# A two-stage feed-forward kernel: first stage in four chunks of 512 tokens and one of 256 instead of eight of 288, with shared buffers and reordered product terms

## The chip, the cores and the metric

One core of a Trainium2 chip. The metric is the device time of one execution in microseconds. Three runs of the kernel before gave 835.99, 837.09 and 838.22 us; the median is 837.09.

## The reference

2304 tokens (4 batches of 576) go through three parts:

```python
attn = softmax(block-causal(q k^T / 8)) v        # 4 batches, 8 heads, 576 x 64; blocks of 64
x = attn as [2304, 512]
h = x @ w_in                                     # [2304, 2048]
x2 = (h - tanh(h)) @ w_out                       # first FFN, [2304, 512]
do = x2 @ w_skip > 0
e = argmax(x2 @ w_gate); gate = softmax weight of e      # 8 experts
out = x2;  out[do] += gate * (relu(x2 @ w1[e]) @ w2[e])  # w1: 512 x 1024, w2: 1024 x 512
```

Every product of the two FFNs is made in float32r from a high and a low part of each operand: high x high, high x low and low x high, so three matmuls stand for one.

## The kernel before

The five engines run hand-written instruction streams that meet by semaphores. PE multiplies, ACT and DVE empty PSUM, SP and POOL issue DMAs.

**Attention** (16 pairs of heads) leaves its output transposed in `x_t`: 128 feature rows, tokens along the free axis, one stretch of 576 per head pair. Meanwhile POOL splits `w_in` into `wi_hi` and `wi_lo`; after attention it splits `w_out` (`wo_hi`, `wo_lo`).

**First FFN.** `each_chunk` (L322) runs `chunk` on PE, ACT and DVE for `NCH` = 8 chunks of `CH` = 288 tokens. In a chunk PE's `chunk` (L1335) goes over `FT` = 16 slices f of 128 hidden units. `hidden(c, f)` (L1268) is 12 matmuls (4 feature blocks x 3 terms) into one of two PSUM banks `h_ps[f % 2]`; `output(c, f-2)` (L1281) is 12 matmuls into the four banks `acc_ps`. All of them are issued by the helper `three` (L1262, so the trace shows L1265), with 128x128 weights and 288 moving columns. The order is hidden(f), output(f-2), hidden(f+1), output(f-1), and at the end output(14), output(15) with no `hidden` between.

For each f ACT takes the tanh (L698, into `tanh_h`), DVE subtracts (`g`, L966), rounds to `g_hi` (L970) and makes `g_lo` (L972). `hidden(f+2)` waits for `g` of f (its bank), `output(f)` waits for `g_hi` and `g_lo` of f. The tanh of f waits for h and for `g` of f-2. `g_hi` of f waits until output(f-2) is done. At the end of a chunk ACT rounds the next chunk's x to `x_hi` (`split_x`), DVE makes `x_lo` (L844), and ACT empties `acc_ps` into `x2_t` (L718).

**Routing of chunk c-1** lies in chunk c: on PE `logits` (12 matmuls, L1301) at f = 2, `turn_rows` (4 transposes, L1309) for the `NR` = 3 row tiles of `RT` = 96 tokens, `rank` (L1316, L1317) at f = 5; on DVE `choose` after f = 3 and `place_tokens` after f = 6. In the last chunk DVE also runs `order_experts` after f = 7 and `order_tiles` after f = 8, which make the order of the experts (`order`, L938) and the places of the first three tiles (`early_base`, L951); after L952 SP loads the first expert's weights and POOL gathers three early tiles (`rec_early`, then `xg_first` to `xg_third`, L517 to L524).

**Second FFN.** 15 tiles of 128 tokens, each of one expert. For a tile k PE runs `turn_he` (8 transposes, L1390), the `first_product` of the next tile (24 matmuls of 512 columns, moving operand `we`), `turn_gathered` (4 transposes, L1328) and `second_product` (24 matmuls of 512 columns into `y_ps`). ACT and DVE split what PE wrote into high and low (`out_xe`, `low_xe`, `out_ht`, `low_ht`). DVE's `mix` (L1058) then makes `y_rows` from `y_ps`; it waits for `y_done` and for `y_free`. There is one `y_rows`. POOL's stream for a tile is serial:

```python
            def put(k, rows):
                wait_apart(pool, y_ready, k + 2)
                pool.indirect_dma_start(out=out, ..., in_=y_rows[:], ...).then_inc(y_out, 16)
                wait_apart(pool, y_out, 16 * k + 16)
                pool.sem_inc(y_free, 1)
```

It fetches the next tile's records (L537), copies them (L542), gathers rows (L544), keeps a copy of both (L555, L556), copies the row numbers (L568), writes `y_rows` out (`put`, L560), waits until that has landed, and only then raises `y_free`. The first step of this stream waits for `base_ready`, which DVE raises at the end of `bases` (L1010).

At the seam PE runs first_product(0) for one bank, logits and turn_rows of the last chunk, the other bank, rank, and so on (L1404 to L1417); ACT and DVE have `high_pieces` and `low_first` (L1071) of the first weights between their steps, and `first_product(0)` waits for `first_columns`, the first four low pieces.

Of the kernel before, what the change touches and what calls it, by code (L numbers as in the profile page):

```python
# [16 lines left out]
F32 = mybir.dt.float32  # L17
# [7 lines left out]
P = 128  # L25


def routed_transformer_block(
# [14 lines left out]
    R_STEPS, R_ONE_HOT = 15, 9  # L43
# [8 lines left out]
    CH = SEQ // 2  # L52
    NCH = TOK // CH
    RT = 96
    NR = CH // RT
# [3 lines left out]
    EARLY, O_HALF = 3, 11  # L59
# [7 lines left out]
    assert FAR > SLOTS and CH % RT == 0 and KC * F1 // DM == PAIRS == FT and F2 == 2 * DM  # L67
# [69 lines left out]
    WORK_AT = CONST_AT + 6144  # L137
# [16 lines left out]
    x_t = sb("x_t", [P, PAIRS * SEQ], F32)  # L154
# [28 lines left out]
    xg_third = sb("xg_third", [P, DM], F32)  # L183
    sb = placer(WORK_AT)
    x_hi, x_lo = sb("x_hi", [P, KC, CH], F32R), sb("x_lo", [P, KC, CH], F32R)
# [3 lines left out]
    x2_rows = sb("x2_rows", [RT, NR, DM], F32)  # L189

# [38 lines left out]
    tab_free, tab_through = sb("tab_free", [1, NE, 2], I32), sb("tab_through", [1, NE, 2], I32)  # L229
    he_hi = sb("he_hi", [P, F2T, P], F32R)  # L230
    x_keep = sb("x_keep", [P, RING, DM], F32)
    sb = placer(RAW_AT)
    xg_early = [sb("xg_first", [P, DM], F32), sb("xg_second", [P, DM], F32), xg_third]
# [11 lines left out]
    with ctx:  # L245
# [18 lines left out]

        CONSTS = 11
# [33 lines left out]
        first_columns = sem("first_columns")  # L299
# [21 lines left out]

        def each_chunk(eng, chunk):  # L322
            chunk(0, first=True, last=False)
            with eng.Fori(1, NCH - 1) as c:
                chunk(c, first=False, last=False)
            chunk(NCH - 1, first=False, last=True)

# [18 lines left out]
        def _(sp):  # L346
# [35 lines left out]
            def store_rows(c):  # L382
                for t in range(NR):
                    wait_apart(sp, x2_rows_done, NR * c + t + 1)
                    sp.dma_start(rows_out[NR * c + t], x2_rows[:, t, :]).then_inc(rows_stored, 16)
                wait_apart(sp, rows_stored, 16 * NR * (c + 1))
                sp.sem_inc(rows_free, 1)
# [26 lines left out]
            store_rows(NCH - 1)  # L414
# [8 lines left out]
        def _(pool):  # L423
# [71 lines left out]
            def list_tokens(c):  # L495
                wait_apart(pool, rec_ready, c + 1)
                for t in range(NR):
# [4 lines left out]
                wait_apart(pool, listed, 16 * NR * (c + 1))  # L502
# [3 lines left out]
            for i in range(EARLY):  # L506
# [4 lines left out]

            pool.wait_ge(early_zero, EARLY)
            pool.wait_ge(rows_stored, 16 * NR * (NCH - 1))
            pool.wait_ge(order_ready, 1)
# [4 lines left out]
            for i in range(EARLY):  # L519
                pool.indirect_dma_start(  # L520
                    out=xg_early[i][:], out_offset=None, in_=out[0:TOK - CH],
                    in_offset=bass.IndirectOffsetOnAxis(ap=rec_early[:, i, 0:1].bitcast(U32), axis=0),
                    bounds_check=TOK - CH - 1, oob_is_err=False,
# [4 lines left out]
            list_tokens(NCH - 1)  # L528
# [3 lines left out]
            pool.wait_ge(rows_stored, 16 * NR * NCH)  # L532
# [62 lines left out]
        def _(act):  # L595
# [21 lines left out]
            def many_x(u):  # L617
                act.wait_ge(many_done, u + 1)
                high(x_t[:, u * SEQ + BLK * FEW:(u + 1) * SEQ], o_many).then_inc(many_out, 1)

            def few_x(u):
                act.wait_ge(few_done, u + 1)
                high(x_t[:, u * SEQ:u * SEQ + BLK * FEW], o_few).then_inc(few_out, 1)
# [34 lines left out]
            def x_of(c, kk):  # L658
                return x_t[:, bass.ds(c * CH + (c // 2) * (PPB - 1) * SEQ + kk * SEQ, CH)]

            def split_x(c):
                for kk in range(KC):
                    high(x_hi[:, kk, :], x_of(c, kk)).then_inc(xc_hi, 1)
# [29 lines left out]
            def chunk(c, first, last):  # L693
# [10 lines left out]
                if not last:  # L704

                    split_x(c + 1)
                else:
# [4 lines left out]
                    act.wait_ge(w_ready, 2)  # L712
                    high_pieces(1, range(0, 2))
# [747 lines left out]
```

## Time and profile before

| | |
|---|---|
| median of 3 runs | 837.09 us (835.99 to 838.22) |
| profiled execution, its own time | 837.9 us |
| its span, first to last instruction | 836.3 us |
| busy: PE / PE weight load / DVE / ACT / POOL | 814.9 / 702.1 / 472.8 / 317.2 / 252.8 us |
| mean granted PE clock | 0.995 |
| attention | until 198.8 us |
| first FFN, first to last matmul | 198.8 to 637.7 us |
| second FFN | from 638.4 us to the end |

Matmuls are pipelined: each is shown as busy from its start until its result is out, so consecutive ones overlap and their busy times sum to more than the time that passed. What a matmul costs in a stream is the distance between two starts.

### The profile page before, as it was taken

Reading aid. Unit: us, or ns where it says so; the run is one execution under the profiler, and the core shown is the slowest. Engines: PE = TensorE matmul, PEld = TensorE weight load, DVE = VectorE, ACT = ScalarE, POOL = GpSimd, SP = SyncE. Lnnn points to the kernel's source line nnn. Section 1 sums busy time; section 2 is a strip of 40 time slices with the busy share of each in tenths; the row PEclk is TensorE's granted clock in tenths of the full one; section 3 lists DMA queues with packets and bytes.
Section 4 is the critical chain, followed back from the end, with each engine's and each line's share of the span. In section 5 each row is a group of like instructions: output and inputs, shape, how many; then the busy total and the mean of one; then the engine's idle time right before and its main releaser. Section 6 shows DMA issues by size and latency. Waiting matters only on the chain.

```text
span 836.3 us, 18439 instructions
## 1 busy us (share of the span) xinstructions
PE 814.9 (97%) x5980; PEld 702.1 (84%) x5981; DVE 472.8 (57%) x1244; ACT 317.2 (38%) x831; POOL 252.8 (30%) x313
## 2 busy tenths in 40 slices
PE   6999999997999999999999999999999999999996
PEld 3555555556999999999999999999998888888885
DVE  4888878785645444344444443544466746556653
ACT  3767667673112121121121211212115435545642
POOL 3766776776820100101001010010030333333333
PEclk9999999998999999999999999999999999999999
DMA  8244444422400000000000000000034176755654
GB/s 172 73 112 99 96 98 101 109 54 63 115 14 10 21 0 28 0 0 28 0 19 9 0 28 0 2 27 1 24 120 134 36 243 215 239 177 181 209 197 143
DMA packets 83006, 66.83 MB, mean 80 GB/s; under 512 B 62970, under 2 KB 62970, under 8 KB 82960
## 3 DMA queue, kind: packets, MB, share of 16 engines
q1 hardware_dynamic: 77824, 60.56, 25.2%
q0 software_dynamic: 3952, 5.38, 2.0%
q8 instruction: 27, 0.44, 0.3%
q10 hardware_dynamic: 1184, 0.30, 0.2%
q14 instruction: 19, 0.16, 0.1%
HBM read 60.59 MB, written 8.83 MB: 83 GB/s over the span
## 4 chain that ended last, share of the span: by engine, by line
PE 92%; DVE 3%; DMA 2%; issue 1%; ACT 1%; POOL 1%; SPq 0%; DVEq 0%; POOLq 0%
PE psum L1265 66%; PE psum L1173 6%; PE psum L1195 6%; PE psum L1144 6%; PE psum L1129 2%; DMA w_half<-in_moe_w_dram 2%; PE psum L1301 2%; PE psum L1390 2%; PE psum L1309 1%; PE psum L1328 1%; DVE neg_max L796 1%; DMA q_rows<-in_q_dram 1%; DVE x_lo L844 1%; POOL probs L474 0%; DVE pt L790 0%
## 5 line engine op out<-in xcount | busy, mean ns | idle before, releaser
L698 ACT ACTIVATE tanh_h<-psum 128x288 f32<-128x288 f32 x128 | 52.6, 411 | 312.7 <-PE psum L1265 304.3
L1265 PE MATMUL psum<-x_hi,wi_hi 128*128 128x288 f32 x512 | 154.9, 303 | 2.5 <-ACT x_hi L597 1.6
L1265 PE MATMUL psum<-x_lo,wi_hi 128*128 128x288 f32 x512 | 152.2, 297 | 0.0
L1265 PE MATMUL psum<-x_hi,wi_lo 128*128 128x288 f32 x512 | 151.7, 296 | 0.0
L1265 PE MATMUL psum<-g_hi,wo_hi 128*128 128x288 f32 x512 | 150.9, 295 | 0.0
L1265 PE MATMUL psum<-g_hi,wo_lo 128*128 128x288 f32 x512 | 150.8, 294 | 0.0
L1265 PE MATMUL psum<-g_lo,wo_hi 128*128 128x288 f32 x512 | 150.6, 294 | 0.0
L966 DVE TENSOR_TENSOR g<-psum,tanh_h 128x288 f32<-128x288 f32 x128 | 58.5, 457 | 141.6 <-ACT tanh_h L698 137.8
L498 POOL DMA_INDIRECT lists<-rec,slot_i x24 | 23.9, 995 | 366.3 <-DVE slot_i L901 318.4
L474 POOL TENSOR_SCALAR probs<-probs,row_inv 128x384 f32<-128x384 f32 (+2 forms) x96 | 98.0, 1031 | 59.5 <-DVE row_inv L803 59.5
L1265 PEld LDWEIGHTS psum<-x_hi,wi_hi 128*128 128x128 f32 x512 | 96.9, 189 | 3.4 <-issue 3.4
L1265 PEld LDWEIGHTS psum<-x_hi,wi_lo 128*128 128x128 f32 x512 | 97.3, 190 | 0.0
L1265 PEld LDWEIGHTS psum<-x_lo,wi_hi 128*128 128x128 f32 x512 | 97.3, 190 | 0.0
L1265 PEld LDWEIGHTS psum<-g_hi,wo_lo 128*128 128x128 f32 x512 | 96.1, 188 | 0.0
L1265 PEld LDWEIGHTS psum<-g_lo,wo_hi 128*128 128x128 f32 x512 | 96.1, 188 | 0.0
L1265 PEld LDWEIGHTS psum<-g_hi,wo_hi 128*128 128x128 f32 x512 | 96.1, 188 | 0.0
L970 DVE CAST g_hi<-g 128x288 fp32r<-128x288 f32 x128 | 43.3, 338 | 79.5 <-PE psum L1265 76.6
L614 ACT ACTIVATE probs<-psum,neg_max 128x576 f32<-128x576 f32 (+2 forms) x144 | 74.6, 527 | 21.5 <-DVE neg_max L796 18.6
L1265 PE MATMUL psum<-we,he_hi 128*128 (+1 forms) x240 | 76.2, 399 | 2.0 <-DVE he_lo L1048 1.9
L992 DVE TENSOR_TENSOR we<-w_half,we x96 | 58.9, 685 | 33.4 <-ACT we L597 33.4
L1265 PE MATMUL psum<-we,xe_hi 128*128 (+1 forms) x240 | 75.5, 396 | 0.8 <-DVE xe_lo L1041 0.5
L796 DVE TENSOR_REDUCE neg_max<-psum 128x1 f32<-128x576 f32 (+2 forms) x144 | 62.9, 484 | 18.0 <-PE psum L1173 17.9
(195 smaller groups left out, 1306.5 us busy)
## 6 DMA issues: line engine op xcount, KB each, us to landing
w_half<-in_moe_w_dram SPq DMA_DIRECT2D x64, 512.0 KB
q_rows<-in_q_dram SPq DMA_DIRECT2D x32, 144.0 KB, 3.0
out_dram<-x_rows SPq DMA_DIRECT2D x24, 192.0 KB, 2.1
k_rows<-in_k_dram SPq DMA_DIRECT2D x30, 144.0 KB, 3.4
v_rows<-in_v_dram SPq DMA_DIRECT2D x32, 128.0 KB, 2.3
w_raw<-in_moe_w_in_dram SPq DMA_DIRECT2D x16, 256.0 KB, 3.4
w_raw<-in_moe_w_out_dram SPq DMA_DIRECT2D x16, 256.0 KB, 2.6
v_rows<-in_v_dram SPq DMA_DIRECT2D x32, 16.0 KB, 2.2
```

What stands on the lines that cost most here:

```text
L474: pool.tensor_scalar(p, p, row_inv[:, j, m:m + 1], None, ALU.mult).then_inc(short_normed, 1)
L498: pool.indirect_dma_start(out=lists, out_offset=bass.IndirectOffsetOnAxis(ap=slot_i[:, t:t + 1].bitcast(U32), axis=0), in_=rec[:, t, :], i ...
L614: act.activation(probs[:, PROB_AT[i]:PROB_AT[i] + BLK * (i + 1)], scores(i), ACT.Exp, bias=neg_max[:, i:i + 1], accum_out=row_sum[:, j, m: ...
L698: act.activation(tanh_h[:, f % 2, :], h_ps[:, f % 2, 0:CH], ACT.Tanh).then_inc(tanh_done, 1)
L796: dve.tensor_reduce(neg_max[:, i:i + 1], scores(i), AX_X, ALU.max, negate=True).then_inc(maxed, 1)
L966: dve.tensor_tensor(g[:, f % 2, :], h_ps[:, f % 2, 0:CH], tanh_h[:, f % 2, :], ALU.subtract).then_inc(g_done, 1)
L970: dve.tensor_copy(g_hi[:, f % 2, :], g[:, f % 2, :]).then_inc(g_hi_done, 1)
L992: ins = dve.tensor_tensor(lo, w_half[:, bass.ds(h % 2, 1), cols].rearrange("p o n -> p (o n)"), hi, ALU.subtract)
L1144: last = pe.transpose(bank[0:width, P * m:P * m + P], probs[:, at:at + width], ident[:] if i == STEPS[j][0] else swap[:])
L1173: mm = pe.matmul(scores(i)[BLK * g:BLK * g + BLK, lo:hi], qt[own, u % 2, BLK * i:BLK * i + BLK], kt[own, u % 2, lo:hi], start=True, stop=T ...
L1195: mm = pe.matmul(dst[own, :], v_rows[0:k, u % 2, c, own], pt[0:k, u % 2, at:at + step * (n - 1) + 1:step, own], start=first, stop=last, sk ...
L1265: mm = pe.matmul(dst, w, m, start=(first and n == 0), stop=(last and n == 2), skip_group_check=True)
```

## The change

`CH` becomes 512 and `NCH` 5, the last chunk has `REST` = 256 tokens; a row tile has 128 tokens (`RT`), so there are 4 in a chunk and 2 in the last. `x_t` is laid out by token, so that a chunk may cross a batch. `x_lo` lies over `x_t`, `tanh_h` is gone (tanh is written into `g`), and `g_lo` lies over `g`. The four last instructions that make `order` move from `order_tiles` to `order_experts`, and `order_ready` is raised there; POOL waits for a new `early_ready`. In both products of the second FFN all terms with a high stationary half come first, and the wait for the low halves is behind them. The splitting of weight half 1 at the seam is moved behind the last chunk's x2.

```diff
-    CH = SEQ // 2
-    NCH = TOK // CH
-    RT = 96
-    NR = CH // RT
+    CH = 512
+    NCH = -(-TOK // CH)
+    REST = TOK - CH * (NCH - 1)
+    RT = P
+    NR, NR_REST = CH // RT, REST // RT
...
-    tanh_h, g = sb("tanh_h", [P, 2, CH], F32), sb("g", [P, 2, CH], F32)
-    g_hi, g_lo = sb("g_hi", [P, 2, CH], F32R), sb("g_lo", [P, 2, CH], F32R)
+    g = sb("g", [P, 2, CH], F32)
+    g_hi = sb("g_hi", [P, 2, CH], F32R)
+    g_lo = placer(G_AT)("g_lo", [P, 2, CH], F32R)
+    x_lo = placer(XT_AT)("x_lo", [P, KC * TOK], F32R)
...
# ACT, chunk
-                        act.wait_ge(g_done, FT * c + f - 1)
-                    act.activation(tanh_h[:, f % 2, :], h_ps[:, f % 2, 0:CH], ACT.Tanh).then_inc(tanh_done, 1)
+                        act.wait_ge(g_used, FT * c + f - 1)
+                    act.activation(g[:, f % 2, 0:n], h_ps[:, f % 2, 0:n], ACT.Tanh).then_inc(tanh_done, 1)
...
# ACT, end of the last chunk
                     high_pieces(0, range(0, PIECES, 2))
                     out_xe(0)
-                    act.wait_ge(w_ready, 2)
-                    high_pieces(1, range(0, 2))
...
# DVE, chunk
-                    if not (first and f < 2):
-                        dve.wait_ge(g_used, n - 2)
-                    dve.tensor_copy(g_hi[:, f % 2, :], g[:, f % 2, :]).then_inc(g_hi_done, 1)
+                    dve.tensor_copy(g_hi[:, f % 2, 0:w], g_f).then_inc(g_hi_done, 1)
...
# PE, first_product
-                pe.wait_ge(xe_low, k + 1)
+                pe.wait_ge(xe_out, k + 1)
                 for n in parts:
...
+                    for kk in range(KC):
+                        for part in range(2):
+                            pe.matmul(dst, xe_hi[:, kk, :], weights(h, part, F2 * kk + 512 * n), ...)
+                    if n == parts[0]:
+                        pe.wait_ge(xe_low, k + 1)
+                    for kk in range(KC):
+                        mm = pe.matmul(dst, xe_lo[:, kk, :], weights(h, 0, F2 * kk + 512 * n), ...)
...
# PE, second_product: the same with he_hi, he_lo; the wait
-                pe.wait_ge(ht_low, 2 * k + 2)
+                    if t % 4 == 0:
+                        pe.wait_ge(ht_out, 2 * k + t // 4 + 1)
```

Three places in the order of the instructions. On ACT in the first FFN, the tanh of the first chunk, its waits, the next chunk's `x_hi` and the emptying of `acc_ps` (written `x_t`, since `x2_t` has the same tile name in the trace's view of it), before:

```order
L698 ACTIVATE tanh_h<-psum 128x288 [waits h_done] x2
L698 ACTIVATE tanh_h<-psum 128x288 [waits g_done,h_done] x14
L597 ACTIVATE x_hi<-x_t 128x288 x4
L597 ACTIVATE x_t<-psum 128x288 [waits g_used]
L597 ACTIVATE x_t<-psum 128x288 x3
```

and now:

```order
L735 ACTIVATE g<-psum 128x512 [waits h_done] x2
L735 ACTIVATE g<-psum 128x512 [waits g_used,h_done] x14
L631 ACTIVATE x_hi<-x_t 128x512 x4
L631 ACTIVATE x_t<-psum 128x512 [waits g_used]
L631 ACTIVATE x_t<-psum 128x512 x3
```

The tanh now waits for the product that reads the same buffer two steps back, and each instruction takes 512 columns.

On DVE in the last chunk, from `o_pos` to `order`, before:

```order
L929 TENSOR_REDUCE o_pos<-o_pm 1x8 [waits o_step]
L966 TENSOR_TENSOR g<-psum,tanh_h 128x288 [waits tanh_done,o_step]
L970 CAST g_hi<-g 128x288 [waits g_used,g_done]
L972 TENSOR_TENSOR g_lo<-g,g_hi 128x288 [waits g_hi_done]
L935 TENSOR_TENSOR o_pm<-o_pos,tile_j 1x64
L936 TENSOR_TENSOR o_pp<-o_pm,code 1x64 [waits o_step]
L937 TENSOR_REDUCE o_code<-o_pp 1x8 [waits o_step]
L938 TENSOR_SCALAR order<-o_code 1x8 [waits o_step]
```

and now:

```order
L973 TENSOR_REDUCE o_pos<-o_pm 1x8 [waits o_step]
L974 TENSOR_TENSOR o_pm<-o_pos,tile_j 1x64 [waits o_step]
L975 TENSOR_TENSOR o_pp<-o_pm,code 1x64 [waits o_step]
L976 TENSOR_REDUCE o_code<-o_pp 1x8 [waits o_step]
L977 TENSOR_SCALAR order<-o_code 1x8 [waits o_step]
L1012 TENSOR_TENSOR g<-psum,g 128x256 [waits o_step,tanh_done]
L1014 CAST g_hi<-g 128x256 [waits g_done]
```

The three instructions with `g` no longer stand between `o_pos` and `order`.

On PE, the last `second_product` of the program, before:

```order
L1390 MATMUL psum<-ident,he 128x128 x3
L329 ISA
L329 TENSOR_LOAD tab_p
L329 ISA x2
L1395 ISA
L1397 REGISTER_ALU [waits ht_low,w_split]
L1265 ISA [waits y_ready]
L1265 MATMUL psum<-we,he_hi 128x512
L1265 ISA
L1265 MATMUL psum<-we,he_hi 128x512
L1265 MATMUL psum<-we,he_lo 128x512
```

and now:

```order
L1447 REGISTER_ALU [waits w_split]
L1452 ISA [waits ht_out,y_ready]
L1452 MATMUL psum<-we,he_hi 128x512
L1452 ISA
...
L1452 MATMUL psum<-we,he_hi 128x512
L1452 ISA [waits ht_out]
L1452 MATMUL psum<-we,he_hi 128x512
...
L1452 MATMUL psum<-we,he_hi 128x512
L1457 MATMUL psum<-we,he_lo 128x512 [waits ht_low]
L1457 MATMUL psum<-we,he_lo 128x512 x3
L1457 MATMUL psum<-we,he_lo 128x512 [waits ht_low]
L1457 MATMUL psum<-we,he_lo 128x512 x3
```

The first matmul no longer waits for `ht_low`; the low terms stand last, behind waits of their own.

## Rows read from the trace of the kernel before

**Rows 1.** Windows: length, busy us of PE, PEld, DVE, ACT, POOL, granted clock, DMA share, GB/s.

```profile
200.00:210.00 10.00, 9.32 (x51) 8.99 (x52) 7.09 (x11) 1.23 (x3) 8.36 (x9) 0.71 0.40 105
620.00:680.00 60.00, 58.90 (x356) 51.81 (x355) 34.13 (x98) 22.93 (x47) 14.45 (x21) 1.00 0.46 140
720.00:760.00 40.00, 40.00 (x195) 33.15 (x194) 24.58 (x40) 21.69 (x42) 13.95 (x24) 1.00 0.54 180
```

**Rows 2.** PE timeline in the first FFN (start us, length us, engine, line, operation; one count).

```profile
205.96 0.29 PE L1265 MATMUL psum<-x_hi,wi_lo 128*128 128x288 f32 x1
...
260.30 2.13 PE L1301 MATMUL psum<-w_route,x_t 128*96 128x9 f32 x24
...
262.28 0.38 PE L1265 MATMUL psum<-x_hi,wi_hi 128*128 128x288 f32 x1
...
265.55 0.60 PE L1309 MATMUL psum<-ident,x_t 128*96 128x128 f32 x4
...
265.91 0.38 PE L1265 MATMUL psum<-x_hi,wi_hi 128*128 128x288 f32 x1
```

**Rows 3.** PE timeline in one tile of the second FFN.

```profile
698.93 1.04 PE L1390 MATMUL psum<-ident,he 128*128 128x128 f32 x8
...
700.95 0.39 PE L1265 MATMUL psum<-we,xe_lo 128*128 x1
...
705.03 0.40 PE L1265 MATMUL psum<-we,xe_lo 128*128 x1
...
706.17 0.39 PE L1265 MATMUL psum<-we,he_lo 128*128 x1
...
711.02 0.39 PE L1265 MATMUL psum<-we,he_lo 128*128 x1
```

**Rows 4.** Start of the first FFN: PE and DVE timeline.

```profile
198.84 0.41 PE L1265 MATMUL psum<-x_hi,wi_hi 128*128 128x288 f32 x1 [1.56 <-ACT x_hi L597]
...
198.18 4.20 DVE L844 TENSOR_TENSOR x_lo<-x_t,x_hi 128x288 fp32r<-128x288 f32 x4 [2.51 <-ACT x_hi L597]
```

**Rows 5.** Groups of instructions, shapes apart: count, busy us, mean ns, idle before.

```profile
L1048 DVE TENSOR_TENSOR he_lo<-psum,he_hi 128x512 fp32r<-128x512 f32 x30 | 19.3, 686 | 0.8 <-ACT he_hi L597 0.6 <-DVE tab_through L1034 0.2
L597 ACT ACTIVATE he_hi<-psum 128x512 fp32r<-128x512 f32 x30 | 16.3, 596 | 46.2 <-PE psum L1390 43.9 <-issue 2.3
```

**Rows 6.** Last chunk: DVE timeline around order_tiles, and the DMA queue of SP.

```profile
613.48 0.20 DVE L935 TENSOR_TENSOR o_pm<-o_pos,tile_j 1x64 f32<-1x64 f32 x1
...
617.04 0.46 DVE L966 TENSOR_TENSOR g<-psum,tanh_h 128x288 f32<-128x288 f32 x1
...
617.74 16.93 SPq L404 DMA_DIRECT2D w_half<-in_moe_w_dram  x8
```

**Rows 7.** The seam: PE and DVE timeline.

```profile
638.35 0.70 PE L1265 MATMUL psum<-we,xe_hi 128*128 128x512 f32 x2 [0.45 <-DVE xe_lo L1041]
...
650.03 0.69 PE L1265 MATMUL psum<-we,xe_hi 128*128 128x512 f32 x2
...
657.13 0.17 DVE L1010 TENSOR_SCALAR tab_base<-c_b 1x29 int32<-1x29 f32 x1
```

**Rows 8.** The tail: timeline of ACT, PE and DVE.

```profile
822.90 1.09 ACT L597 ACTIVATE he_hi<-psum 128x512 fp32r<-128x512 f32 x2 [2.99 <-PE psum L1390]
...
825.22 0.73 PE L1265 MATMUL psum<-we,he_hi 128*128 x2 [1.92 <-DVE he_lo L1048]
...
831.45 0.75 DVE L1058 SCALAR_TENSOR_TENSOR y_rows<-psum,rec_keep,x_keep 128x512 f32<-128x512 f32 x1 [6.63 <-PE psum L1265]
```

**Rows 9.** POOL timeline in the second FFN.

```profile
659.45 0.60 POOL L537 DMA_DIRECT2D rec_ahead<-lists  x1 [5.66 <-issue]
...
703.71 1.04 POOL L560 DMA_INDIRECT out_dram<-y_rows,rec_now  x1 [1.09 <-issue]
...
827.81 1.04 POOL L560 DMA_INDIRECT out_dram<-y_rows,rec_now  x1 [1.10 <-issue]
...
830.96 0.19 POOL L568 COPY rec_now<-rec_keep 128x1 int32 x1 [2.12 <-DMA out_dram<-y_rows,rec_now]
```

More of the change, by code:

```diff
@@ L493, in _, with list_tokens @@
             pool.sem_inc(rec_free, 1)
-            def list_tokens(c):
+            def list_tokens(c, last=False):
+                n = row_tiles(last)
                 wait_apart(pool, rec_ready, c + 1)
-                for t in range(NR):
+                for t in range(n):
                     pool.indirect_dma_start(
@@ L691, in _, with chunk @@
             split_x(0)
-            def chunk(c, first, last):
+            def chunk(c, first, last, to_rest=False):
+                n = tokens(c, last)
                 for f in range(FT):
@@ L880, in choose @@
+                step(dve.tensor_reduce(r_arg[:, now], r_tmp[:, now, :], AX_X, ALU.max))
+                step(dve.tensor_tensor(r_one[:, now, :], each(code[:], n), wide(r_arg[:, now], n), ALU.is_equal))
+                step(dve.tensor_scalar(r_sel[:, now], skip, 0.0, None, ALU.is_gt))
+                step(dve.tensor_tensor(r_one[:, now, :], r_one[:, now, :], wide(r_sel[:, now], n), ALU.mult))
+                for t in range(n):
                     step(dve.tensor_tensor(r_sofar[:, t + 1, :], r_sofar[:, t, :], r_one[:, t, :], ALU.add))
@@ new lines, in choose, with place_tokens @@
+                dve.tensor_copy(rec[:, now, 0], tok_f[:, now])
+            def place_tokens(c, last=False):
+                n = row_tiles(last)
+                now = slice(0, n)
+                step = stepper(R_STEPS * c + 8 + n)
+                dve.wait_ge(ranked, c + 1)
+                rank = route_ps[0:RT, RANK_AT:RANK_AT + n * NE].rearrange("p (t n) -> p t n", t=n)
+                step(dve.tensor_tensor(r_tmp[:, now, :], rank, each(list_at[:], n), ALU.add))
+                step(dve.tensor_tensor(r_tmp[:, now, :], r_tmp[:, now, :], r_one[:, now, :], ALU.mult))
+                step(dve.tensor_reduce(r_slot[:, now], r_tmp[:, now, :], AX_X, ALU.add))
+                step(dve.scalar_tensor_tensor(r_slot[:, now], r_sel[:, now], -float(FAR), r_slot[:, now], ALU.mult, ALU.add))
+                if not last:
+                    dve.tensor_copy(r_sofar[:, 0, :], r_sofar[:, NR, :])
+                    dve.tensor_scalar(tok_f[:], tok_f[:], float(CH), None, ALU.add)
+                dve.tensor_scalar(slot_i[:, now], r_slot[:, now], float(FAR), None, ALU.add).then_inc(rec_ready, 1)
@@ L1266, in three, with hidden @@
                 return mm
-            def hidden(c, f, first):
+            def hidden(c, f, first, last):
+                w = tokens(c, last)
                 if not (first and f < 2):
@@ L1333, in turn_early, with chunk @@
                 turn_xe(i, xg_early[i])
-            def chunk(c, first, last):
+            def chunk(c, first, last, to_rest=False):
                 for f in range(FT):
-                    hidden(c, f, first)
+                    hidden(c, f, first, last)
                     if f >= 2:
-                        output(c, f - 2, first)
+                        output(c, f - 2, first, last)
                     if not first:
@@ L1348, in chunk @@
                             count(r_sofar[:, NR, :], counted_early)
[L1349 removed]
+                output(c, FT - 2, first, last)
                 if last:
                     turn_early(0)
[L1352 removed]
+                output(c, FT - 1, first, last)
             pe.wait_ge(raw_used, PAIRS)
```

246 lines of the change are left out of this document (132 added, 114 removed).

## The prediction

> **What bounds the kernel now.** I read the table of windows first: PE is busy for nearly all of the windows at 620 and 720 us, at the full clock (1.00), while DVE, ACT and POOL are busy for little more than half or less, and the DMA engines for 54% at 720 [rows 1]. Busy time of pipelined matmuls doesn't say what one costs, so the next view is PE's timeline, read by starts.
>
> In the first FFN the starts are evenly spaced: from 205.96 to 260.30 us there are 409 matmuls of 288 columns, 0.1329 us each [rows 2]. 288 columns at 2.4 GHz are 0.1200 us, so 0.0129 us comes on top, and there are no holes. In the second FFN 18 matmuls of 512 columns lie between 700.95 and 705.03, 0.2267 us each (0.2133 for the columns, 0.0134 on top). In `second_product` 21 lie between 706.17 and 711.02, 0.2310 us each [rows 3]. So the addition hardly depends on the number of columns, and fewer, wider matmuls pay it less often. That is what the first FFN can win.
>
> The second FFN has a second chain beside PE. PE's tile takes 12.32 us (698.93 to 711.25, one matmul behind the last row) [rows 3]. POOL's writes of results go from 703.71 to 827.81 in ten tiles, 12.41 us each [rows 9]: POOL's serial stream (fetch, gather, copy, write, wait for landing) is as long as PE's tile. It starts at 659.45, 2.3 us after DVE has made the bases at 657.13 [rows 7, 9]. At the end the last write but one has landed at 830.96 (POOL goes on), and the last `mix` starts at 831.45 [rows 8, 9]. It waits for both that landing and PE's product (825.22 + 24 x 0.231 + 0.3 for the last one to come out = 831.1), and they come within about 0.1 us of each other.
>
> **The first FFN, product by product.**
> Before: 8 chunks x 384 = 3072 matmuls x 0.1329 = 408.3 us. After: 4 x 384 = 1536 of 512 columns and 384 of 256. I take 0.2267 for 512 columns, since the addition it implies (0.0134) is nearest to the one measured in this very loop (0.0129); the other end is 0.2310. For 256 columns I take the 288-column price less 32 columns, 0.1329 - 0.0133 = 0.1196. Its bounds are 0.109, the distance of transposes that load 128 columns of weights (1.04 us for eight, the last one about 0.27) [rows 3], and 0.1329. Sum: 1536 x 0.2267 + 384 x 0.1196 = 348.2 + 45.9 = 394.1. **Gain 14.2 us.** With 0.2310 it is 7.6. The 256-column bounds move it by +4.1 or -5.1.
>
> The Trainium skill (TensorE: Matmul & The Clock Gate, "Back-to-back issue gap") gives N/2.4 + 2.5 ns. By it the products would take 376 us before and 373 after, a gain of 3 instead of 14. The rows disagree with its 2.5 ns: 12.9 and 13.4 are measured here, and they decide.
>
> **Routing on PE.** `logits` takes 262.28 - 260.30 = 1.98 us a chunk, in 24 passes of 0.083 us with 96 columns of weights. `turn_rows` takes 0.36 and the first matmul behind such a change another 0.08, together 0.44 [rows 2]. Row tiles fall from 24 to 18, so `logits` has 72 instead of 96 matmuls, but with 128 columns of weights. If a pass cost the same, this would win 4 us. In proportion to the weight columns a pass costs 0.110, and the transposes with 128 columns stand at 0.109 [rows 3]. I take 0.110 and so no gain; 4 us stays as a bound. The Trainium skill (same page, "LDWEIGHTS (loading the stationary operand)") has a load as columns / 1.2 ns, 80 and 107 ns; the 96-column row agrees. Transposes stream 128 columns either way: 6 fewer, 2.6 us. `rank`, about 0.36 with its change, goes from 8 to 5: 1.1 us. About 3.2 us of these 3.7 lie in chunks other than the last. But four chunks' `logits` of 3.6 us now lie inside the first FFN instead of seven of 2.06 (14.4 both times), and the last one's at the seam is 1.8 against 2.0. I book **2.6 us inside the first FFN** and 0.6 at the seam.
>
> **New waits in the first FFN.**
> - The tanh of f now waits until output(f-2) is done. It then has 24 matmuls (5.4 us) until `hidden(f+2)` needs g. Tanh and g take 0.60 and 0.69 at 512 columns by the groups of that width [rows 5], with the hand-over about 1.5 us. Hidden. Were PE not to cover it, it would cost 1.5 us for each of 80 slices. What is late next is f = 15, where output(14) and output(15) follow each other: tanh, g, g_hi, g_lo need about 0.2 + 0.6 + 0.7 + 0.45 + 0.7 = 2.7 us against 12 matmuls, 2.7 us. I book 0.3 us for all of them.
> - Start of the last chunk: ACT empties four banks of 512 columns (about 2.3 us) before the first tanh. `hidden(2)` would start 24 x 0.1196 = 2.9 us after the chunk's start and gets its bank at 3.4: **0.55 us**.
> - Last chunk, DVE: `order_tiles` took 617.04 - 613.48 = 3.56 us for 18 steps, 0.2 each [rows 6]. `order_experts` grows to 15 steps (3.0 us), `order_tiles` shrinks to 14 (2.7). A slice is now 2.9 us, so DVE falls behind over slices 7 and 8, and `hidden(11)` waits **0.57 us**.
> - `x_lo` of the first chunk took 4.20 us for four beside POOL's splits [rows 4]. They are wider now, but so is what PE does meanwhile. The loss at the start (24 matmuls in 7.12 us instead of 3.19, clock 0.71 in that window [rows 1]) stays as it is, give or take 0.6.
> - `w_half`: before, the issues begin at 617.74 and go on for 16.9 us [rows 6], to 3 us ahead of PE's end. Now `order` is ready about 31 us into the last chunk instead of 34, and the chunk is 2 us shorter; so the weights land at about the same distance from PE's end, and the wait for half 1 stands further behind it. Early gather: ready about 0.6 us before PE wants it; up to 1 us of wait is in the range.
>
> First FFN: 14.2 + 2.6 - 0.3 - 0.55 - 0.57 = **15.4 us shorter**.
>
> **The seam.** Before, 12.3 us pass from the end of the first FFN (637.7) to `first_product(1)` at 650.03 [rows 7]. Step by step with the new streams: the start waits for `first_columns`, 1.15 us (0.6 before), since the last tanh is later against PE's end; then the stall of 0.35 us before the second half goes, a row tile and 0.6 us go. About 11.35, **0.95 us less on PE**. But DVE's own stream to `base_ready` (four more steps of splitting ahead of it) gets no shorter: 20.2 us behind the end of the first FFN against 19.6 (657.3). POOL's stream so starts **0.6 us later**, reckoned from that end.
>
> **The second FFN's reorder.** In the loop PE has no wait that it could remove: the starts are evenly spaced through every tile. At the tail PE waits 1.92 us for `he_lo` and starts at 825.22 [rows 8]; with the high terms first it starts after one `out_ht` (822.90 and 0.6), at about 823.65, **1.6 us earlier**. Both this and the seam's 0.95 us are gains of PE alone. The last `mix` also waits for POOL's landing, which moves with POOL's start and comes 0.6 us later. So 0.95 + 1.6 us are hidden and the end comes about **0.4 us later** against the end of the first FFN.
>
> **Sum:** -15.4 + 0.4 = -15.0 us against the profiled execution, 837.9 (span 836.3): 822.9. That execution lies 0.8 above the median of 837.09, so the forecast for the median is **822.1 us**.
>
> **Rivals.**
> - *POOL doesn't end last.* For it: in the profile the two releasers of the last `mix` tie within 0.1 us, and POOL's distances vary. Against: its mean distance is above PE's, and PE gets 2.5 us ahead. Then 0.95 + 1.6 + 0.4 more are won: 819.1.
> - *Wide matmuls at 0.2310.* For it: half of the 512-column ones do that, all with weights from `he_hi` and `he_lo`. Against: the first FFN's addition is the small one in all its products. 6.6 us less gain: 828.7.
> - *The row tiles are cheaper* than in proportion: 4 us more at most, 818.
> - *Slower: PE loses its clock at new waits.* At the start of the first FFN a stop of 1.56 us and the gaps behind it go with the clock at half and cost 3.9 us [rows 1, 4]. The change makes waits at four chunk ends, twice in the last chunk and at the seam. If each cost 3.9 us, seven would cost 27 us and the kernel would take 849; from four on it is slower than before. Against: these waits are under 1.2 us, and around the seam, where PE stops for 0.45 us [rows 7] and is busy for 58.90 of 60, the clock stays at 1.00 [rows 1].
> - *The change does nothing*: that the matmuls' addition grew with their width would do it; the rows at 512 exclude that.
>
> **Chances.** Forecast (POOL last, 0.2267; 820.5 to 824.5) 0.48; POOL not last or cheaper row tiles 0.25; 0.2310 or another loss of up to 7 us 0.22; more loss, still faster, 0.02; within 0.3% (2.5 us, about what a measurement can tell from no change) 0.01; slower by the clock 0.02. The range takes the second and third cases with their bounds: 816 to 829 us.
>
> **What would show it.** In the first FFN, starts 0.2267 and 0.1196 us apart, chunks of about 93 us. `logits` 3.5 us. In the last chunk two waits of about 0.6 us. At the tail PE starts on `ht_out`, and the last `mix` starts when the last write but one has landed, well after PE's last matmul. The forecast is wrong if the distance is 0.231, if PE shows waits inside the big chunks, or if `mix` starts 0.4 us after PE's end.

## The result and the profile after

| | before | changed |
|---|---|---|
| median | 837.83 us | **843.45 us** |
| runs | 10, 835.99 to 842.07 | 10, 842.68 to 847.72 |
| profiled execution, time / span | 837.9 / 836.3 us | 847.7 / 846.1 us |
| mean granted PE clock | 0.995 | 0.984 |
| first FFN ends (last start and one distance) | 637.7 us | 649.4 us |
| from there to the end of the span | 198.6 us | 196.7 us |

The kernel is slower by 0.65%: the ratio to before is 1.0065, with an interval from 1.0049 to 1.008. The forecast was a gain, 822.1 us, range 816 to 829. The profiled execution lies 4.3 us above its kernel's median; the last sections come back to that. The last two lines of the table say where to look: everything that was lost was lost in the first FFN.

There the chain of waits of the changed kernel, from the row work of one chunk to the next, shows both losses at once (columns: start us, length us, what):

```profile
299.62 3.47 PE psum L1345 x32
303.09 7.19 PE psum L1308 x24
310.28 0.44 PE psum L1353 x4
310.71 5.48 PE psum L1308 x24
...
316.77 0.60 ACT x_rows L631
...
317.42 0.66 PE psum L1353 x4
318.07 5.49 PE psum L1308 x24
```

Twenty-four matmuls of 512 columns take 5.48 us at 310.71 and at 318.07. The same number takes 7.19 at 303.09, right behind `logits`. And ahead of the transposes of `turn_rows` (L1353) the chain leaves PE and goes through ACT, which it does nowhere in the first FFN of the kernel before. Two timelines show that stop from both sides, first PE's (columns: start, length, engine, line, operation, output and inputs, count, idle time and releaser):

```profile
315.79 0.39 PE L1308 MATMUL psum<-g_hi,wo_lo 128*128 128x512 f32 x1
317.42 0.66 PE L1353 MATMUL psum<-ident,x_t 128*128 128x128 f32 x4 [1.24 <-ACT x_rows L631]
```

then ACT's:

```profile
316.28 0.60 ACT L735 ACTIVATE g<-psum 128x512 f32<-128x512 f32 x1 [2.80 <-PE psum L1308]
316.77 0.59 ACT L631 ACTIVATE x_rows<-psum 128x512 f32<-128x512 f32 x1
```

The last matmul of `output(f-2)` starts at 315.79. Only behind it may the tanh go (316.28); behind the tanh, on the same engine, stands the copy of a turned row tile (316.77); and only behind that copy may PE turn the next row tile (317.42), which is the very next thing in PE's stream. That copy could have run 6 us earlier: the transposes that it reads started at 310.28. It was ready and stood in ACT's queue behind a tanh that waited.

The second loss is in the table of windows (length, busy us of PE, PEld, DVE, ACT and POOL, granted clock, DMA share, GB/s), which answers to [rows 1]:

```profile
300.00:310.00 10.00, 10.00 (x52) 8.64 (x52) 1.81 (x3) 0.31 (x1) 0.00 (x0) 0.83 0.00 0
310.00:320.00 10.00, 8.76 (x44) 6.99 (x43) 6.09 (x21) 1.91 (x4) 0.00 (x0) 1.00 0.07 26
400.00:410.00 10.00, 10.00 (x50) 8.59 (x51) 1.39 (x3) 0.39 (x1) 0.00 (x0) 0.83 0.00 0
500.00:510.00 10.00, 10.00 (x39) 8.32 (x39) 0.69 (x1) 0.00 (x0) 0.00 (x0) 0.66 0.01 2
595.00:615.00 20.00, 17.95 (x126) 17.55 (x126) 6.90 (x27) 2.36 (x6) 0.00 (x0) 0.83 0.08 27
```

PE is busy in all of 500 to 510 and yet gets through 39 matmuls, at a granted clock of 0.66. The window from 310 to 320, which holds a stop of PE, is at 1.00. PE's timeline shows where in the window the clock was low:

```profile
497.73 0.39 PE L1308 MATMUL psum<-g_hi,wo_lo 128*128 128x512 f32 x1
497.95 4.04 PE L1345 MATMUL psum<-w_route,x_t 128*128 128x9 f32 x32
501.85 0.78 PE L1308 MATMUL psum<-x_hi,wi_hi 128*128 128x512 f32 x1
...
503.27 0.63 PE L1308 MATMUL psum<-x_hi,wi_hi 128*128 128x512 f32 x1
503.70 0.63 PE L1308 MATMUL psum<-x_lo,wi_hi 128*128 128x512 f32 x1
...
508.14 0.40 PE L1308 MATMUL psum<-g_hi,wo_hi 128*128 128x512 f32 x1
508.38 0.40 PE L1308 MATMUL psum<-g_lo,wo_hi 128*128 128x512 f32 x1
```

Up to 497.73 starts are 0.227 us apart, the 2.4 GHz level. Then PE runs 32 matmuls of 9 columns for about 3.9 us. That is longer than the 3.47 us of the first chunk, because the clock had fallen before the stretch was over (its passes slow down on the way, as they also do in the last chunk). Behind it the starts are 0.43 apart, which is 512 columns at the 1.2 GHz level; by 508.14 they are 0.24 apart and soon 0.227 again. PE did not stop in between.

At the seam and at the tail the kernel does in the main what was forecast (PE and DVE timelines, then the tail's; they answer to [rows 7 to 9]):

```profile
649.26 0.28 PE L1308 MATMUL psum<-g_hi,wo_lo 128*128 128x256 f32 x1
650.19 2.11 PE L1427 MATMUL psum<-we,xe_hi 128*128 128x512 f32 x8 [0.65 <-DVE we L1119]
...
660.48 2.08 PE L1427 MATMUL psum<-we,xe_hi 128*128 128x512 f32 x8
```

```profile
668.49 0.17 DVE L1054 TENSOR_SCALAR tab_base<-c_b 1x29 int32<-1x29 f32 x1
```

```profile
833.17 3.91 PE L1452 MATMUL psum<-we,he_hi 128*128 x16 [0.54 <-DVE y_rows L1102]
...
836.92 1.98 PE L1457 MATMUL psum<-we,he_lo 128*128 x8
837.17 1.03 POOL L594 DMA_INDIRECT out_dram<-y_rows,rec_now  x1 [1.10 <-issue]
841.32 0.75 DVE L1102 SCALAR_TENSOR_TENSOR y_rows<-psum,rec_keep,x_keep 128x512 f32<-128x512 f32 x1 [7.16 <-POOLq L599]
```

PE's last matmuls are done at 838.9, and the last `mix` starts at 841.32, released by POOL's queue and not by PE. So POOL's serial stream ends the kernel. One thing at the tail is not as forecast: PE's last product starts at 833.17, released not by ACT's copy (`ht_out`) but by DVE's `mix` of the tile before, 0.1 us later.

### The profile page after: what moved, and what is told of

It is laid out like the page before. It is cut to its first block, busy times and chain, and to the rows that moved or that the text cites. A ratio compares the mean times of both kernels' runs of the same rounds, so it can differ in the third digit from the quotient of the medians.

```text
span 846.1 us, 14981 instructions
## 1 busy us (share of the span) xinstructions
PE 807.9 (95%) x4744; PEld 629.1 (74%) x4745; DVE 436.9 (52%) x1026; ACT 303.0 (36%) x750; POOL 251.3 (30%) x307
## 4 chain that ended last, share of the span: by engine, by line
PE 79%; DMA 9%; issue 4%; DVE 3%; POOL 2%; ACT 2%; POOLq 1%; ACTq 0%; DVEq 0%
PE psum L1308 46%; PE psum L1238 6%; PE psum L1216 6%; PE psum L1187 6%; DMA xg<-out_dram,rec_next 5%; DMA out_dram<-y_rows,rec_now 3%; PE psum L1427 3%; PE psum L1172 2%; PE psum L1452 2%; PE psum L1345 2%; PE psum L1432 2%; PE psum L1353 1%; PE psum L1457 1%; ACT x_rows L631 1%; POOL rec_next L576 1%
## 5 line engine op out<-in xcount | busy, mean ns | idle before, releaser
L1012 DVE TENSOR_TENSOR g<-psum,g 128x512 f32<-128x512 f32 (+1 forms) x80 | 51.0, 638 | 270.1 <-ACT g L735 269.8
L1308 PE MATMUL psum<-g_hi,wo_hi 128*128 128x512 f32 (+1 forms) x320 | 118.9, 371 | 0.4 <-DVE g_lo L1016 0.3
L1308 PE MATMUL psum<-g_lo,wo_hi 128*128 128x512 f32 (+1 forms) x320 | 118.4, 370 | 0.0
L1308 PE MATMUL psum<-g_hi,wo_lo 128*128 128x512 f32 (+1 forms) x320 | 118.1, 369 | 0.0
L1308 PE MATMUL psum<-x_hi,wi_hi 128*128 128x512 f32 x256 | 104.5, 408 | 2.8 <-DVE x_lo L881 2.7
L1308 PE MATMUL psum<-x_lo,wi_hi 128*128 128x512 f32 (+1 forms) x256 | 102.3, 400 | 0.0
L1308 PE MATMUL psum<-x_hi,wi_lo 128*128 128x512 f32 x256 | 102.2, 399 | 0.0
L831 DVE TENSOR_REDUCE neg_max<-psum 128x1 f32<-128x576 f32 (+2 forms) x144 | 63.0, 484 | 17.4 <-PE psum L1216 17.3
L631 ACT ACTIVATE we<-w_half (+1 forms) x112 | 60.1, 620 | 31.8 <-PE psum L1432 27.7
L1216 PE MATMUL psum<-kt,qt 64*64 64x64 f32 (+7 forms) x640 | 59.8, 435 | 1.3 <-ACT probs L648 0.7
L1308 PEld LDWEIGHTS psum<-x_hi,wi_lo 128*128 128x128 f32 x256 | 49.6, 194 | 10.9
```

The costliest lines, as they stand in the source:

```text
L631: return act.activation(dst, src, ACT.Copy)
L831: dve.tensor_reduce(neg_max[:, i:i + 1], scores(i), AX_X, ALU.max, negate=True).then_inc(maxed, 1)
L1012: dve.tensor_tensor(g_f, h_ps[:, f % 2, 0:w], g_f, ALU.subtract).then_inc(g_done, 1)
L1216: mm = pe.matmul(scores(i)[BLK * g:BLK * g + BLK, lo:hi], qt[own, u % 2, BLK * i:BLK * i + BLK], kt[own, u % 2, lo:hi], start=True, stop=T ...
L1308: mm = pe.matmul(dst, w, m, start=(first and n == 0), stop=(last and n == 2), skip_group_check=True)
```

## The experiments

Two losses stood out in this reading, and each had a theory. **Theory 1**: PE stops because the copy of the row tiles now stands behind a tanh that waits (three stops in each of four chunks). **Theory 2**: apart from that, the clock falls behind `logits`, whose stretch has grown from 2.0 to 3.5 us and more. The **rival** to theory 2 is the one on record, "PE loses its clock at new waits": the stops themselves make the clock fall, so removing them gives both back. Another candidate is that the wide matmuls themselves bring the clock down. In what follows the unchanged kernel's median is the one taken beside each experiment. The changed kernel was timed on another occasion, so a difference to it is given in medians, and beside it as the ratios to before give it.

**The copy ahead of the tanh.** In the changed kernel ACT's copy of a row tile moves in front of the tanh of the same slice:

```diff
                 for f in range(FT):
+                    if 4 <= f < 4 + NR and not first:
+                        rows(c - 1, f - 4)
                     act.wait_ge(h_done, FT * c + f + 1)
...
-                    if 4 <= f < 4 + NR and not first:
-                        rows(c - 1, f - 4)
```

> The changed kernel, but ACT copies a row tile out (x_rows) ahead of the tanh of the same slice instead of behind it. Theory 1: PE stops at turn_rows 1 to 3 of every chunk because the copy it waits for stands behind a tanh that itself now waits for output(f-2); each stop costs 1.39 us in the big chunks (nine) and 1.18 in the last (three), 16.0 us in all. Expected then: no PE idle at the transposes, about 16 us less than the changed kernel, so some 827 to 828 us against 837.5 before. Rival: the tanh itself, wider and later, is what PE is short of (then hidden or output take over the wait, and less than 5 us are won). Second rival, on the clock: if the half clock in the first FFN comes from these stops and not from logits, it goes here too, and it is over 19 us less.

Measured: 827.96 us (827.9 to 830.74), before 838.84, ratio 0.988 with an interval from 0.9841 to 0.9918. Against the changed kernel's median that is 15.5 us less (15.5 by the ratios). The chain no longer goes through ACT; the stops are gone. Windows of this kernel:

```profile
300.00:320.00 20.00, 20.00 (x100) 17.03 (x100) 7.91 (x24) 2.66 (x6) 0.00 (x0) 0.91 0.07 26
400.00:410.00 10.00, 10.00 (x44) 8.15 (x44) 3.74 (x15) 1.31 (x3) 0.00 (x0) 0.92 0.01 5
580.00:600.00 20.00, 20.00 (x148) 20.00 (x147) 6.96 (x27) 3.32 (x9) 0.00 (x0) 0.83 0.11 41
```

PE is busy in all 20 us of 580 to 600, without a stop, and the clock still comes out at 0.83. The rival falls for the first FFN: the clock goes down with no stop near it, and the gain is not the 19 us and more that the rival wanted.

**`logits` in two lots.** In the changed kernel, two row tiles at f = 1 and two at f = 2, so that no stretch of narrow matmuls is longer than 1.7 us:

```diff
-                for t in range(row_tiles(last)):
+                for t in tiles or range(row_tiles(last)):
...
-                        if f == 2:
-                            logits(c - 1)
+                        if f in (1, 2):
+                            logits(c - 1, tiles=range(2 * f - 2, 2 * f))
...
```

> The changed kernel, but the 16 logits matmuls of a chunk in the first FFN come in two lots of 8, behind hidden(1) and behind hidden(2)/output(0), instead of all at once; the stops at turn_rows stay. Theory 2: 3.5 us of 9-column matmuls in one stretch are what makes the clock fall behind them (granted clock 0.66 in the 10 us from 500 of the profiled execution). Expected then: no window in the first FFN behind its start under 0.95, mean clock 0.994 or more, 3 to 9 us less than the changed kernel, about 838. Rival: the stops at turn_rows bring the clock down, and then it is still under 0.99 on average and the time is within 1.5 us of the changed kernel.

Measured: 837.28 us (836.26 to 838.32), ratio 0.9975 (0.9954 to 0.9996); 6.2 us less than the changed kernel (7.5 by the ratios). The stops are left in, and the clock is at its full level in all four places:

```profile
300.00:320.00 20.00, 18.77 (x95) 15.52 (x95) 7.91 (x24) 2.51 (x5) 0.00 (x0) 1.00 0.03 13
400.00:410.00 10.00, 10.00 (x52) 8.43 (x53) 4.10 (x9) 1.03 (x3) 0.00 (x0) 1.00 0.00 0
500.00:510.00 10.00, 10.00 (x48) 8.24 (x47) 4.15 (x18) 0.83 (x2) 0.00 (x0) 1.00 0.01 2
580.00:600.00 20.00, 18.98 (x152) 18.35 (x151) 8.10 (x31) 4.60 (x11) 0.00 (x0) 1.00 0.00 1
```

The group of the row transposes in the same kernel (columns: count, busy us, mean ns, idle before and releaser) still carries nearly the whole first loss (14.2 us idle; counted from start to start, the same twelve stops are 16.0):

```profile
L1354 PE MATMUL psum<-ident,x_t 128*128 128x128 f32 x64 | 10.3, 283 | 14.2 <-ACT x_rows L631 14.2
```

So the two losses are independent, and each has its own cause.

**Both.** The two edits together:

> Both edits together on the changed kernel. Theories 1 and 2 together: 16 plus 3 to 9 us less than the changed kernel, 819 to 825 us, which is the blind forecast's 822; mean clock 0.994 or more; 384 matmuls of 512 columns plus about 5.9 us per big chunk, 93 us. If something else were lost in the first FFN beside the two, it stays above 826.

Measured: 820.55 us (819.33 to 822.95), ratio 0.979 (0.9752 to 0.9828), mean clock 0.998 in the profiled execution and 0.994 or 0.995 in the other three. 22.9 us less than the changed kernel, against 15.5 + 6.2 = 21.7 for the two apart (by the ratios 23.0, against 15.5 + 7.5 = 23.0). Its chain of waits, at the place of the first fence above:

```profile
293.23 1.69 PE psum L1345 x16
294.91 5.60 PE psum L1308 x24
300.51 1.69 PE psum L1345 x16
302.20 5.60 PE psum L1308 x24
...
326.40 51.71 PE psum L1308 x228
```

The chain stays on PE through the whole chunk, 228 matmuls take 51.71 us, 0.2268 each, and a big chunk takes 93.3 us as expected. The price of the split is one more change between kinds of work on PE: the 24 matmuls behind a lot take 5.60 us, against 5.48 elsewhere, now twice in a chunk instead of once; and the two lots together take 3.4 us against 3.47 in one. That comes to less than 0.1 us a chunk.

**The wait alone, in the kernel before.** The tanh waits for `output(f-2)` there too, and nothing else is changed:

```diff
-                        act.wait_ge(g_done, FT * c + f - 1)
+                        act.wait_ge(g_used, FT * c + f - 1)
```

> The kernel before with one line of the change: the tanh of f waits until output(f-2) is done (g_used) instead of until g of f-2 is made. Chunks of 288, all buffers separate. Theory 1: PE now stops at turn_rows 1 and 2 of seven chunks for tanh 0.41 + copy 0.58 + hand-overs 0.2 = 1.2 us each, 14 to 17 us more than before, 852 to 854. Rival (the width of the chunk is what makes the stop): within 3 us of before.

Measured: 860.04 us (858.39 to 864.64), before 838.84, ratio 1.0259 (1.0208 to 1.031): 21.2 us more. PE's timeline shows the same stop in chunks of 288 columns, and another at the end of a chunk:

```profile
269.03 0.29 PE L1265 MATMUL psum<-g_hi,wo_lo 128*128 128x288 f32 x1
270.36 0.64 PE L1309 MATMUL psum<-ident,x_t 128*96 128x128 f32 x4 [1.04 <-ACT x_rows L597]
...
309.42 0.29 PE L1265 MATMUL psum<-g_hi,wo_lo 128*128 128x288 f32 x1
310.12 0.38 PE L1265 MATMUL psum<-g_hi,wo_hi 128*128 128x288 f32 x1 [0.40 <-DVE g_lo L972]
```

Starts are 1.33 us apart instead of 0.13: 1.20 us lost, two in each of seven chunks, 16.8 us. The second kind, at f = 15, is 0.70 less 0.13, 0.56 us in seven chunks, 3.9. Together 20.7 of the 21.2 measured. The expectation had left the second kind out. One line is enough to make this kernel 2.6% slower, without wide chunks and with the mean clock at 0.993.

**`logits` twice, in the kernel before.** Each group of narrow matmuls is issued twice into the same place, which gives a stretch as long as that of the wide chunks with nothing else changed (the routing work on PE is done twice):

```diff
-                for t in range(NR):
+                for t in [*range(NR), *range(NR)]:
```

> The kernel before with every logits group issued twice in a row (same result): 24 matmuls and 3.96 us in one stretch instead of 12 and 1.98. If only its own time counts: 8 x 1.98 = 15.8 us more than before, clock 0.995 as before. Theory 2: a stretch of that length brings the clock down behind it in some or most chunks, as in the changed kernel: mean clock 0.990 or less, 18 to 35 us more than before, and windows with a clock under 0.95 behind logits. Rival: it is the width of the chunk (512 columns, 128 weight columns) or the row stops that bring it down, and the clock holds here.

Measured: 868.53 us (868.21 to 871.69), before 839.53, ratio 1.0344 (1.0315 to 1.0372), 29.0 us more; mean clock 0.974. PE's timeline:

```profile
260.16 4.17 PE L1301 MATMUL psum<-w_route,x_t 128*96 128x9 f32 x48
264.18 0.38 PE L1265 MATMUL psum<-x_hi,wi_hi 128*128 128x288 f32 x1
...
266.72 0.44 PE L1265 MATMUL psum<-g_hi,wo_hi 128*128 128x288 f32 x1
266.96 0.44 PE L1265 MATMUL psum<-g_lo,wo_hi 128*128 128x288 f32 x1
```

The stretch is 4.0 us instead of 2.0 [rows 2], and behind it 288-column matmuls start 0.24 us apart, the 1.2 GHz level, before they come back to 0.133. Two more microseconds in each of eight chunks explain about 16 of the 29. The other 13 are put down to the clock by subtraction; the profile bears it out, since the 24 matmuls behind the stretch take 4.5 to 5.8 us in each of the seven chunks instead of 3.28. Wide matmuls fall as a cause too: the chunks are narrow here, no copy waits, and the clock goes down all the same.

**The new order of terms, alone, in the kernel before.** Only the second FFN's two products put the high halves first:

```diff
-                pe.wait_ge(ht_low, 2 * k + 2)
...
+                    if t % 4 == 0:
+                        pe.wait_ge(ht_out, 2 * k + t // 4 + 1)
```

> The kernel before with only the reordered terms of the two products of the second FFN and their waits. Theory (of the prediction): PE starts its last second_product some 1.6 us earlier, but the last mix waits for POOL's last write but one to land, so the time stays within 0.7 us of before (ratio 0.999 to 1.001), and the last mix starts more than 1 us behind PE's last matmul. Rival: the end follows PE, 1.6 to 2 us less (0.998).

Measured: 840.03 us (836.61 to 842.41), before 839.53, ratio 0.9999 (0.9983 to 1.0016). The tail:

```profile
830.79 2.00 PE L1412 MATMUL psum<-we,he_lo 128*128 x8
...
833.98 0.75 DVE L1058 SCALAR_TENSOR_TENSOR y_rows<-psum,rec_keep,x_keep 128x512 f32<-128x512 f32 x1 [6.01 <-POOLq L565]
```

PE is done at 832.8, 1.2 us ahead of the `mix`, which waits for POOL. In the kernel before the two came together [rows 8, 9]. So the end follows POOL and the time is the same, as forecast. But this profile has a loss of its own at the seam (PE timeline; count and idle time as above):

```profile
641.98 2.21 PE L1301 MATMUL psum<-w_route,x_t 128*96 128x9 f32 x24 [1.24 <-ACT x_t L597]
...
645.03 3.33 PE L1381 MATMUL psum<-we,xe_hi 128*128 128x512 f32 x8
```

PE starts the first product earlier, so it stops ahead of `logits` instead, for 1.24 us; behind that stop and 2.0 us of narrow matmuls the granted clock is 0.50 from 644.3 to 647.6, and the bases come at 659.25, 21.4 us behind the end of the first FFN instead of 19.4. Nine of the twelve executions have a mean clock of 0.992 or less, against six of the seventeen of the kernel before. Whether a small gain of the reorder is eaten by the clock here is therefore open.

**The old order of terms in the repaired kernel.** The reverse of that experiment, from the kernel with both repairs:

> The repaired kernel (copy ahead of the tanh, logits in two lots) with the three terms again in the old order and the old waits. Theory: at the tail PE's last product starts 1.6 us later, but the last mix was held by POOL anyway (812.84 against PE's end near 811.1), so it costs 0.3 us there and up to 0.6 at the seam: 0 to 1.2 us more than the repaired kernel. Rival: the reorder carries the gain, 2.5 us or more are lost.

Measured: 822.86 us (822.12 to 823.71), ratio 0.9805 (0.9781 to 0.9828). That is 2.3 us above the repaired kernel's 820.55, but the ratios' intervals overlap, and the repaired kernel's own executions span 3.6 us. A small gain of the new order is possible there and not shown.

**One gather less at the tail.** Since POOL ends last, the last round of its loop need not fetch records that nobody uses. In the repaired kernel:

```diff
-            with pool.Fori(0, last_tile) as j:
+            with pool.Fori(0, last_tile - 1) as j:
                 fetch_next(j + 3)
                 store(j)
+            store(last_tile - 1)
             store(last_tile)
...
```

> The repaired kernel, and POOL leaves out its last gather, of a tile that nobody reads, so that the last write but one is issued some 7 us earlier. Theory: the last mix then starts 0.4 us behind PE's last product instead of about 1.8, and the end comes 1 to 2 us earlier than in the repaired kernel. Rival: the mix is held by something else, no difference (under 0.5 us).

Measured: 819.01 us (818.3 to 822.36), ratio 0.976 (0.9734 to 0.9786). In the profiled execution (822.36) the last `mix` starts 1.06 us behind PE's last matmuls instead of 1.8, not the 0.4 expected: the last write but one is issued 5.1 us ahead of PE's end instead of 1.4, but takes 6 us to land instead of 3.3.

**The repaired kernel once more**, to see how far 820.55 holds on another occasion:

> The repaired kernel (copy ahead of the tanh, logits in two lots) once more, beside the next one on the same chip, so that the two can be told apart: 820 to 822 us, ratio to before 0.977 to 0.981.

Measured: 820.33 us (820.02 to 823.84), before 838.98, ratio 0.9792 (0.9765 to 0.9819).

**One gather less, and the last three steps of `order_tiles` put off.** DVE does them two slices later, so that `hidden(11)` of the last chunk waits less for g:

```diff
+            def order_rest():
+                step = o_stepper(O_HALF + 11)
...
+                    if f == 10 and last:
+                        order_rest()
```

> The repaired kernel without POOL's last gather, and with the last three steps of order_tiles two slices later in the last chunk, so that DVE falls less behind (hidden(11) waited 0.79 us longer than its turn for g). Expected: that wait falls to 0.2 us or less, and both together bring 1.5 to 3 us against the repaired kernel: 818 to 819.5 us. If the early gather, which PE waits for at turn_early, ends last there, the 0.6 us of the split are not seen.

Measured: 820.82 us (818.14 to 824.6), ratio 0.9778 (0.9747 to 0.9809). The wait at `hidden(11)` is gone, and the last `mix` starts 0.4 us behind PE. What is left stands a little later (PE timeline):

```profile
623.39 1.11 PE L1381 MATMUL psum<-ident,xg_first 128*128 128x128 f32 x4 [3.50 <-DMA xg_third<-out_dram,rec_early]
```

Once PE no longer stops for the copies, it reaches the early gather before the gather has landed, and waits: 0.74 us in the first profile of the repaired kernel, 2.15 with one gather less, 3.50 here. (The prediction had allowed up to 1 us.) In the last two profiles the clock also falls at this stop; here it is 0.50 from 622 to 628. The executions of the last three kernels split in the same way. Those with a mean clock of 0.997 or more took 820.0 to 820.3 us (repaired, on its second occasion), 818.3 to 819.0 (one gather less) and 818.1 to 818.8 (both); the others, at 0.992 to 0.995, took 821.6 to 824.6. Compared like with like that looks like a gain of 1 to 2 us, from three executions each, but the medians of all executions don't tell either kernel apart from the repaired one. It is not shown.

The version to keep is the changed kernel with the two repairs: 820.3 to 820.6 us on two occasions, 2.1% faster than before (0.979, by the intervals 1.7 to 2.5%), and 2.7% faster than the change as it was made (820.55 / 843.45).

## Why the prediction was wrong

**Matmul products: right.** The 228 matmuls behind 333.23 in the changed kernel, like those behind 326.40 in the repaired one, are 0.2268 us apart (0.2267 forecast), and the 256-column ones 0.12 (0.1196). The 14 us were there to be won. The Trainium skill (TensorE: Matmul & The Clock Gate, "Back-to-back issue gap") has N/2.4 + 2.5 ns, which it calls the gap of an isolated matmul; this case again gives N/2.4 + 13.5 ns at 512 columns, and the measurement decides.

**Price of the routing work: right in its own time, wrong in what it does.** `logits` takes 3.47 us with the full clock (3.5 forecast), so four chunks' `logits` of 3.6 us against seven of 2.06 was right as a sum. But it was booked as neutral because only the sum was compared; what the stretch does to the clock was put at nothing. A stretch of 2.0 us left the clock alone in the kernel before; one of 3.5 to 4 us did not. In the profiled execution the 24 matmuls behind it took 7.19, 7.01 and 8.39 us instead of 5.5, and 4.96 instead of 2.95 in the last chunk: 8.1 us. The stretches themselves (3.47, 3.64, 3.88, 4.58) and the few matmuls around them cost some 2 more. Over the median executions it is less: 6.2 us by the experiment that splits them (7.5 by the ratios).

**"The tanh of f now waits until output(f-2) is done ... Hidden": this step failed.** It followed the wait in one direction only, from the tanh to g and so to PE, and there it was right. It did not list what stands behind the tanh in ACT's queue. For f = 4 to 7 that is the copy of a row tile, and PE wants it right behind the matmuls that the tanh waits for. The chain closes: PE's last matmul of `output(f-2)`, tanh, copy, transposes on PE. A stop is 1.62 us between two starts where 0.23 is normal, so 1.39, three in each of three big chunks: 12.5. In the last chunk it is 1.18 three times, 3.5. **16.0 us**, where the text booked nothing. The experiment that moves the copy gave 15.5 back, and the one that puts the wait alone into the kernel before cost 21.2 (where there are 14 such stops, and 7 more at f = 15). The text had even named the price of an uncovered slice (1.5 us "for each of 80 slices") and then looked only for slices that g would miss.

**f = 15, start of the last chunk, `hidden(11)`: nearly right.** 0.32 us idle at f = 15, in one chunk only (0.3 booked for all), next to nothing at the start of the last chunk (0.55 booked; the first matmul of `hidden(2)` comes 0.30 us behind the one before it instead of 0.12), and 1.01 us idle at `hidden(11)` (0.57 booked):

```profile
630.04 0.28 PE L1308 MATMUL psum<-g_hi,wo_lo 128*128 128x256 f32 x1
631.34 0.39 PE L1308 MATMUL psum<-rest_hi,wi_hi 128*128 128x256 f32 x1 [1.01 <-DVE g L1012]
```

**The seam and the tail: right in kind, off by 2.3 us in all.** PE's part of the seam took 11.1 us (11.35 forecast); the bases were ready 19.3 us after the first FFN (20.2 forecast); from the end of the first FFN to the end it was 1.9 us shorter where 0.4 longer was forecast. POOL's stream began 1.0 us earlier, not 0.6 later (its first fetch is at 670.11, 1.6 us behind the bases instead of 2.3), and its last write but one came 167.1 us after that instead of 168.4; why is open. That the PE gains of the reorder are hidden behind POOL is what the after profile shows, and the experiment with the reorder alone agrees, with the reserve made there.

**The rival "PE loses its clock at new waits"** had the right sign and the wrong cause. It put the fall at waits. In the first FFN the windows with waits and split `logits` are at 1.00; those without waits and with long `logits` are at 0.83 to 0.92. Its chance of 0.02 was drawn from the seam, where a stop of 0.45 us left the clock alone. Two profiles with a longer stop at the seam are different: with 1.17 us (the wait alone, in the kernel before) and 1.24 us (the reorder alone) the clock fell behind the `logits` that followed. So a stop may well play a part there, which no run separates; it was not what cost the time here. The Trainium skill (same page, "HAM oscillation — how this bites in real kernels") states the rule as "no PE-idle gaps"; here PE had none at `logits`, and the clock fell.

**The sum, again.** First FFN as forecast −15.4, seam and tail −1.9, stops +16.0, clock +10, give +8.7 us against the profiled execution before; 847.7 − 837.9 = 9.8 was measured. Of the 1.1 left over, 0.4 is in the small waits (1.8 counted from start to start, 1.42 booked). The routing work can account for the rest, since it won some 1.1 us instead of the 2.6 booked: beside its products a big chunk of the repaired kernel has 93.3 − 87.1 = 6.2 us, about 25 us in four chunks, against 3.7 us in a chunk of the kernel before, about 26 in seven. In the medians (843.45 − 837.83 = 5.6) the clock weighs less: −17.3 + 16.0 + 6.2 gives +4.9.

## What to carry to other kernels

When a change adds a wait to an instruction, write down everything that stands behind it on that engine and who waits for each of those, before asking whether the instruction's own result comes in time; work that was ready earlier belongs ahead of the wait. When a change makes fewer, larger stages, compare the length of each stretch of narrow matmuls and not only their sum, since the clock held behind stretches of 2.0 us between wide matmuls and fell at 3.5 to 4. Splitting it in two cost less than 0.1 us a chunk here and gave back 6 us in all. And look again behind a repair: once PE was faster, it met a transfer that had been in time before.

## What the runs showed of the hardware

- The granted clock fell to the 1.2 GHz level in or just behind 3.5 to 4.6 us of continuous matmuls of 9 columns, though PE is shown as busy throughout and had been at full clock for tens of microseconds before. In the first FFN it did not fall behind a stretch of 2.0 us or behind two of 1.7 us, in any profile. At the seam it fell in two profiles behind a stretch of 2.0 us that followed a stop of 1.17 or 1.24 us. In the changed kernel it was low from about 501 to 507.8 us, some 6 us of that in wide matmuls.
- How much each fall costs differs from one to the next: 24 matmuls took 7.01, 7.19 and 8.39 us in one execution.
- At the start of the first FFN, behind a stop of 1.9 us for `x_lo`, the clock over 196 to 210 us was 1.00 in one profile of the repaired kernel and 0.88 in the other. Executions of one kernel differ by 3 us or so; this is one place where they do, and the seam is another. At the early gather the clock fell behind stops of 2.15 and 3.50 us and held behind stops of 0.74 to 1.84 us (four profiles). What decides it was not found out.
- A separate buffer for tanh, which might remove the wait and not only its cost, was not tried.
